# Two kinds of VectorE work put between the packed rows and their copy, and epsilon added by a sum over pairs

## The reference, cut to what matters

```python
def sm_attn(qq, kk, vv):
    s = scale * qq @ kk.T
    a = exp(s - max(s))
    a = a / (sum(a) + 1e-09)          # the epsilon of this case
    return a @ vv
packed = sm_attn(p, k, v)             # 32 rows per head
x = sm_attn(q, packed, packed)        # 576 tokens per head, over 32 packed rows
h = x @ w_in                          # 4608 tokens x 512 -> 1024
solu = h * softmax(h)
ln = (solu - mean) / sqrt(var + 1e-06) * g_ln
y = ln @ w_out                        # -> 512
h2 = max(y @ w1, y @ w2, y @ w3)      # -> 768
out = h2 @ w_out2                     # -> 512
```

## Time and profile before

| | |
|---|---|
| median of 3 runs | 1023.25 us |
| profiled execution, its own time | 1022.33 us |
| span from first to last instruction | 1020.5 us |
| TensorE busy | 993.5 us, 97% |
| VectorE busy | 594.0 us, 58% |
| ScalarE busy | 356.0 us, 35% |
| GpSimd busy | 269.4 us, 26% |
| mean granted TensorE clock | 0.998 of full speed |

### The profile page before, as it was taken

One profiled execution on the slowest core, in us unless ns is written; L12 is line 12 of the kernel. 1 busy time (PEld: TensorE's weight loads), 2 busy tenths in 40 slices (PEclk: granted clock), 3 DMA queues, 4 the chain that ended last, 5 costly groups with the idle time before them and its releaser, 6 DMA issues.

```text
span 1020.5 us, 14952 instructions
## 1 busy us (share of the span) xinstructions
PE 993.5 (97%) x6026; PEld 796.6 (78%) x6026; DVE 594.0 (58%) x960; ACT 356.0 (35%) x583; POOL 269.4 (26%) x228
## 2 busy tenths in 40 slices
PE   6989999999999999999999999999999999999998
PEld 5656567887887887878888888888888888888887
DVE  1788899765865767564655726664365736553121
ACT  5867753333442442333212422224122332122111
POOL 0368753439949992700000000000000000000000
PEclk9999999999999999999999999999999999999999
DMA  8979827226564582235745345453544535432341
GB/s 296 390 259 307 295 102 258 106 103 250 216 224 182 193 317 83 103 113 187 295 161 203 134 176 192 174 212 114 196 175 185 179 131 214 163 140 93 117 161 42
DMA packets 49764, 189.85 MB, mean 186 GB/s; under 512 B 9888, under 2 KB 9888, under 8 KB 39328
## 3 DMA queue, kind: packets, MB, share of 16 engines
q1 hardware_dynamic: 43472, 153.89, 42.4%
q0 software_dynamic: 6224, 35.00, 9.1%
HBM read 141.30 MB, written 47.58 MB: 185 GB/s over the span
## 4 chain that ended last, share of the span: by engine, by line
PE 84%; DVE 8%; ACT 4%; issue 3%; DMA 1%; POOL 0%; SPq 0%; ACTq 0%
PE ps L1171 28%; PE ps L783 27%; PE ps L1203 14%; PE ps L1194 5%; PE ps L1073 3%; PE ps L894 2%; DVE h_lo L1574 1%; PE ps L990 1%; DVE spot L1889 1%; PE ps L797 1%; DVE spot L1880 1%; DMA p_raw<-in_p_dram 1%; PE ps L799 1%; DVE a2T L1662 1%; ACT qT L1248 1%
## 5 line engine op out<-in xcount | busy, mean ns | idle before, releaser
L1171 PE MATMUL ps<-ys,slot 128*128 128x512 f32 x1512 | 345.8, 390 | 0.6
L1171 PEld LDWEIGHTS ps<-ys,slot 128*128 128x128 f32 x1512 | 283.2, 188 | 62.5 <-ACT spot L1248 4.0
L1880 DVE TENSOR_TENSOR spot<-ps,spot 128x512 f32<-128x512 f32 x108 | 74.3, 688 | 104.6 <-PE ps L1171 75.1
L1248 ACT ACTIVATE spot<-ps 128x512 f32<-128x512 f32 x90 | 52.8, 597 | 207.9 <-PE ps L1171 196.8
L783 PE MATMUL ps<-ln_lo,w_out_s_hi 128*128 128x512 f32 x280 | 109.2, 390 | 0.0
L783 PE MATMUL ps<-ln_hi,w_out_s_lo 128*128 128x512 f32 x280 | 109.0, 389 | 0.0
L783 PE MATMUL ps<-ln_hi,w_out_s_hi 128*128 128x512 f32 x280 | 108.9, 389 | 0.0
L1203 PE MATMUL ps<-w_out_s_lo,h_hi 128*128 128x512 f32 x216 | 84.0, 389 | 0.0
L1203 PE MATMUL ps<-w_out_s_hi,h_hi 128*128 128x512 f32 x216 | 84.0, 389 | 0.0
L1203 PE MATMUL ps<-w_out_s_hi,h_lo 128*128 128x512 f32 x216 | 84.0, 389 | 0.0
L1390 ACT ACTIVATE u<-ps,neg_max 128x1024 f32<-128x1024 f32 x36 | 40.2, 1117 | 112.7 <-DVE neg_max L1737 112.7
(11 more groups left out here) (160 smaller groups left out, 1504.0 us busy)
## 6 DMA issues: line engine op xcount, KB each, us to landing
slot<-w_operands SPq DMA_DIRECT2D x36, 1792.0 KB, 7.2
w_operands<-stage POOLq DMA_DIRECT2D x18, 1024.0 KB, 4.9
v_raw<-in_v_dram SPq DMA_DIRECT2D x8, 1152.0 KB, 7.1
q_raw<-in_q_dram SPq DMA_DIRECT2D x32, 288.0 KB, 5.3
y_features<-yst SPq DMA_DIRECT2D x9, 1024.0 KB, 4.8
y_raw<-y_features SPq DMA_DIRECT2D x9, 1024.0 KB, 5.2
out_dram<-spot SPq DMA_DIRECT2D x36, 256.0 KB, 2.0
slot<-w_operands SPq DMA_DIRECT2D x9, 1024.0 KB, 5.1
```

Source lines behind the costliest of these rows:

```text
L1171: last = pe.matmul(ps[:, group_bank(g, k), :], w[:, a - 1, i, kk, :], ys[:, b, j, kk, :], start=n < 4 and kk == 0 and e == 0, stop=kk == K ...
L1248: return act.activation(dst, src, ACT.Copy)
L1880: dve.tensor_tensor(dst[:, :], a, b, op).then_inc(ready, 1)
```

## The change

`sum1` and `sum2` get a second column that holds the epsilon, written once at the start; the row sums go to the first column, and the epsilon is added by a reduction over the pair instead of a tensor_scalar. `lo_a(b)` of batches 0 and 1 moves from the end of step b into step b+1, between `take_packed` and `copy_packedT`. The second `centre` of steps 3, 4 and 5 moves to the same place of its own step, ahead of `inverse2(b, 1)` and both `turn_out`.

```diff
-    sum1 = place("sum1", [P, QUADS])
+    sum1 = place("sum1", [P, QUADS, 2])
-    sum2 = place("sum2", [P, QUADS, S // NPACK])
+    sum2 = place("sum2", [P, QUADS, S // NPACK, 2])
+    eps_ready = sem("eps_ready")
...
-                               bias=nb1[:, g:g + 1], scale=SCALE, accum_out=sum1[:, g:g + 1]).then_inc(s1_exp, 1)
+                               bias=nb1[:, g:g + 1], scale=SCALE, accum_out=sum1[:, g, 0:1]).then_inc(s1_exp, 1)
...
             dve.memset(share[:, :], SHARE).then_inc(share_ready, 1)
+            dve.memset(sum1[:, :, 1], SM_EPS).then_inc(eps_ready, 1)
+            dve.memset(sum2[:, :, :, 1], SM_EPS).then_inc(eps_ready, 1)
+            dve.wait_ge(eps_ready, 2)
             dve.wait_ge(gain_loaded, 16)
...
                 dve.wait_ge(s1_exp, QUADS * b + QUADS)
-                dve.tensor_scalar(sum1_eps[:, :], sum1[:, :], SM_EPS, None, ALU.add).then_inc(inv1_step, 1)
+                dve.tensor_reduce(sum1_eps[:, :], sum1[:, :, :], AX.X, ALU.add).then_inc(inv1_step, 1)
...
-                dve.tensor_reduce(sum2[:, g, :], quad(g), AX.X, ALU.add).then_inc(inv2_step, 1)
+                dve.tensor_reduce(sum2[:, g, :, 0], quad(g), AX.X, ALU.add).then_inc(inv2_step, 1)
                 dve.wait_ge(inv2_step, c + 1)
-                dve.tensor_scalar(sum2_eps[:, g, :], sum2[:, g, :], SM_EPS, None, ALU.add).then_inc(inv2_step, 1)
+                dve.tensor_reduce(sum2_eps[:, g, :], sum2[:, g, :, :], AX.X, ALU.add).then_inc(inv2_step, 1)
...
             def step(b, third=True, second=True, first=True):
-                direct = third and b < 2
...
                 if second:
                     take_packed(b + 1)
+                if third and 0 < b < 3:
+                    lo_a(b - 1)
+                elif MEAN_STEP < b < B - 2:
+                    centre(b - MEAN_STEP - 1, 2 * (b - MEAN_STEP - 1) + 1)
                 if third and not first:
                     max_h(0, 1)
                 if second:
                     copy_packedT(b + 1)
...
-                if MEAN_STEP < b < B - 2:
-                    centre(b - MEAN_STEP - 1, 2 * (b - MEAN_STEP - 1) + 1)
                 if third:
                     turn_out(b, 1)
...
-                if direct:
-                    lo_a(b)
```

## The result

The changed kernel took 1017.07 us (median of 5 runs, 1016.94 to 1018.30) against 1022.72 us for the kernel before on the same chip (5 runs, 1021.96 to 1023.51): ratio 0.9950, 95% interval 0.9939 to 0.9962. On a second chip it was 1016.92 against 1023.25: 0.9943, 0.9930 to 0.9955. The forecast was 1017.8 (1016.2 to 1020.6), faster. Medians and intervals leave out two executions of the kernels of the experiments that took 2020.26 and 4927.88 us, far above their neighbours (one in part 2, one in part 3).

The account below looks back on a forecast made before the run. TensorE, busy 97%, was taken as the bound, so gains count only where it waits. Terms 0.67 + 2.20 + 1.30 - 0.68 + 0.41 + 0.33 + 0.26 + 0.93 = 5.42 us, from 1023.25 to 1017.8 (1016.2 to 1020.6).

Parts of the forecast that it names:

- lo_a(0), 0.67 of 1.26: End of step 0: moving it frees 1.26 us of VectorE's queue, of which 0.67 us reaches TensorE.
- lo_a(1), its wait and its hold: Step 2: GpSimd stretches lo_a(1) from 1.35 to 2.90 us; removing TensorE's wait for it brings another 2.20 us.
- The clock, 1.30: Step 2, turn_a1 to pack: with no idle time before, TensorE's half clock goes, another 1.30 us.
- the clock still falls: Rival, 8%: another idle time replaces the one removed, so the gain is 4.1 us, 1019.1 us.
- What is late next, -0.68: Step 2 into 3: GpSimd's backlog delays sub2(2, 0), exp2 and the kT copy for turn_q(3, 0); takes back 0.68 us.
- The new place: lo_a meets GpSimd's scale2: packed copy 0.40 us earlier in step 1, 1.36 us late in step 2 but covered.
- the rival of a partial loss: Rival, 22%: packed copies come later than worked out or step 2's cover shrinks; gain 3.0 us, 1020.2 us.
- the slower one: Rival, 4%: moved instructions queue behind GpSimd's scale2 and the packed copies behind them; 2.7 us slower, 1025.9 us.
- nothing arrives: Rival, 5%: DMA loads set the pace of the attention, steps lengthen at loads, up to the whole gain; 1023 us.
- centre, 0.41 + 0.26: Moving the second centre from between the two turn_out brings 0.41 us in step 3 and 0.26 in step 5.
- epsilon, 0.33 + 0.93: Adding the epsilon by an unheld reduction brings 0.33 us in step 5 and 0.93 in the last step.
- the prediction's sign: In the changed trace, TensorE's wait for u, before at 1.5 us in the last step, is 0.6 us.

Follow-up runs that it names:

- part 2: Against the kernel before: both moves with the epsilon still a tensor_scalar, 1020.49 us; lo_a's move and the epsilon change without centre's move, 1019.05 us.
- part 3: Changed kernel with lo_a and the second centre one place later, behind copy_packedT: 1021.08 us.
- experiment 4: Kernel before with GpSimd's batch-0 remainder held until lo_a(1) is done, 1022.72 us; kernel before with 18 extra TensorE transposes before scores2(2, 1), 1023.01 us.
- Experiment 5's first kernel: Changed kernel with GpSimd's split_merged(0, 1) behind both sub2 of batch 2 instead of in front: 1017.75 us.

## Why the prediction was right, step by step

**lo_a(0), 0.67 of 1.26.** Measured 0.68 and 0.64.

**lo_a(1), its wait and its hold.** `scores2(2, 1)` was forecast 2.87 us earlier by the ruler and came so: 61.12 - 0.56 (the start) - 2.87 = 57.69, measured 57.70. That the hold by GpSimd is what made 1.35 into 2.90 is shown by experiment 4.

**The clock, 1.30.** `turn_a1` to `pack` is 2.09 as forecast, and `pack` 65.19 - 0.56 - 60.47 = 4.16 us earlier (4.17). So 1.30 is right for the place. What it is worth further on is less, and the prediction's own bounds say so: with the half clock kept, `pack`, and `turn_q(3, 0)` behind it, would be 2.87 us earlier, against 3.49 with GpSimd's bound. Within this change the clock then brings 0.62 us (an estimate, from these two bounds), since the other 0.68 is what the backlog takes back. So the rival "the clock still falls", for a fall at this place, was priced 0.7 us too high. In the kernel before the traces give 0.91 at the end (experiment 4), but the executions don't confirm it: the mean granted clock of before was 0.998 in 53 of 63, median 1023.31, and 0.999 or 1.000 in 6, median 1022.40, and these six spread from 1022.02 to 1024.60. By its mean granted clock 1 execution of before in 10 doesn't have the fall that the one trace showed.

**What is late next, -0.68.** `sub2(2, 0)` 60.75 (forecast 60.81, the start taken off), `turn_q(3, 0)` 63.17 (63.28). Experiment 5's first kernel gives 0.63 back when the backlog is moved: its `turn_q(3, 0)` is 4.17 us earlier, as much as the prediction had for `pack`.

**The new place.** The packed copy of step 2 was to be 1.36 us late: it starts at 66.32, and TensorE had been ready at 64.96 (the `turn_packed` of 64.48 takes 0.44), 1.36. Its cover held. The copies behind `centre`, VectorE in steps 3, 4 and 5:

```profile
81.53 0.74 DVE L1590 SCALAR_TENSOR_TENSOR weight_raw<-w_out_raw,gain,column_mean 128x512 f32<-128x512 f32 x1
82.91 0.58 DVE L1631 COPY packedT<-ps 64x128 f32<-64x128 f32 x2 [0.65 <-PE ps L905]
...
96.94 1.00 DVE L1590 SCALAR_TENSOR_TENSOR weight_raw<-w_out_raw,gain,column_mean 128x512 f32<-128x512 f32 x1
98.32 0.58 DVE L1631 COPY packedT<-ps 64x128 f32<-64x128 f32 x2 [0.39 <-PE ps L905]
...
111.97 1.07 DVE L1590 SCALAR_TENSOR_TENSOR weight_raw<-w_out_raw,gain,column_mean 128x512 f32<-128x512 f32 x1
113.36 0.58 DVE L1631 COPY packedT<-ps 64x128 f32<-64x128 f32 x2 [0.32 <-PE ps L905]
```

VectorE still idles 0.65, 0.39 and 0.32 us in front of each copy (forecast 0.6, 0.2, 0.1), so the rival of a partial loss did not occur, nor the slower one, which needs copies late by more than the hole in most of the five steps. For "nothing arrives", a load would have to hold TensorE; none of its waits from 26 to 147 us names one.

**centre, 0.41 + 0.26; epsilon, 0.33 + 0.93.** The first and the last are confirmed one by one: 0.41 in the table at b=5, 0.40 against the kernel without `centre`'s move; 0.91 to 0.94 for the wait for `u`, which is 0.6 us in the kernel run again, as the prediction's sign had it. The two of step 5 add up (0.59 forecast; from b=5 to b=7 the table gives 0.50 and 0.65), but their division was wrong: alone, the epsilon brings 0.03 there, and taking `centre`'s move out of the whole costs 0.60 there and 1.28 in all, not 0.67. That the two sizes of step 5 made up for each other is luck.

**The sentence that failed.** "What the freed stalls are worth: step 3 (0.6) and step 4 (0.7) nothing" is right against the kernel before, and wrong as a price of the edit. It took the stalls of before as given, and didn't ask where the tensor_scalars would stand once the moves had shifted VectorE against GpSimd: 2.12 us in step 3. Without the epsilon's change about 3 of 5.6 us would have been lost again. The sum came out right because it was made for all the parts together.

**The clock in step 7.** The prediction held 1.79 us of idle time to be harmless, since before has such a one with no fall behind it. In the changed kernel's trace:

```profile
136.42 0.27 PE L839 MATMUL ps<-qT,packedT 64*32 64x64 f32 x5 [1.78 <-ACT qT L1249]
...
138.61 1.76 PE L1074 MATMUL ps<-ident,u 128*128 128x128 f32 x8
```

and in the same kernel run again:

```profile
136.27 0.27 PE L839 MATMUL ps<-qT,packedT 64*32 64x64 f32 x5 [1.79 <-ACT qT L1249]
...
137.60 1.09 PE L1074 MATMUL ps<-ident,u 128*128 128x128 f32 x8
```

Eight transposes take 1.76 us behind one and 1.09 behind the other. So the rival "the clock still falls" does occur, elsewhere and in some executions, for 0.75 us. Part of what the slower matmuls take falls into a wait that was there: TensorE's 0.6 us for `u`, which the kernel run again has, is absent in the execution with the fall. By the mean granted clock 2 of 10 executions of the changed kernel have a fall (0.998), too few to move the median.

## What to carry to other kernels

Price several edits of one queue together and in shifted times: here an addition over two elements, worth 0.9 us alone, decided about 3 us of 5.6 (by the ruler). When VectorE is moved against GpSimd, look for every small tensor_scalar, of two elements per partition or more, that will now start inside one of GpSimd's two-input instructions, and make it a reduction if it can be one. Work moved off a path is cheap only in a hole that the engine has anyway; one place later the same instructions cost 3.3 us by the ruler.

## What was not expected of the hardware

**How long GpSimd holds VectorE depends on GpSimd's instruction.** Its two-input TENSOR_TENSOR holds to its end (the rows above). Its one-input TENSOR_SCALAR of 2.77 us holds only at first. GpSimd in step 3 of the changed kernel:

```profile
80.55 2.76 POOL L692 TENSOR_SCALAR m_odd<-merged_first 128x1024 fp32r<-128x1024 f32 x1
```

`centre`, two inputs in SBUF, starts 0.98 us later at 81.53 and takes its normal 0.74. GpSimd in the kernel with both moves:

```profile
58.46 2.77 POOL L691 TENSOR_SCALAR m_even<-merged_first 128x1024 fp32r<-128x1024 f32 x1
```

and VectorE beside it:

```profile
58.55 0.97 DVE L1599 TENSOR_SCALAR sum_eps<-sum 128x2 f32<-128x2 f32 x1 [0.55 <-ACT a L1277]
```

58.55 + 0.97 = 59.52, 1.06 us behind GpSimd's start and 1.71 ahead of its end. The 0.46 us of the earlier trace rows ends at 150.08, 1.07 behind the start of this one in the kernel before:

```profile
149.01 2.77 POOL L658 TENSOR_SCALAR w_out_s_hi<-weight_raw 128x1024 fp32r<-128x1024 f32 x1 [0.64 <-DVE weight_raw L1586]
```

The unheld 1.19 us of the earlier trace rows began 1.64 us into its like the earlier trace rows. So it is about the first microsecond that holds; why, no run here shows.

The whole-length rule weighed in the prediction (the Trainium skill, "SBUF — State Buffer", Who interferes with whom) thus holds for GpSimd's two-input instructions and not for this one, and its 1.0 us in step 3 was not paid. The same section of the Trainium skill says that tensor_reduce never contends for the shared port pair on this chip, while tensor_scalar can. With that the trace agrees: 24 reductions between 156 and 193 ns, none held.

**A tensor_scalar with one element per partition is not held.** The additions that were held have 2 and 18. The one behind each row maximum has one, and this one of the kernel before starts 0.61 us into the GpSimd instruction of 56.70 to 59.06:

```profile
57.31 0.15 DVE L1594 TENSOR_SCALAR nb<-m 128x1 f32<-128x1 f32 x1
```

All 14 of them take 153 to 156 ns. The `lo_a(1)` right behind it, at 57.38, is the one that took 2.90 in place of 1.35 us.

**A clock that falls by chance.** In the profiled executions without added transposes, TensorE's clock went from 1.00 to 0.50 behind 2.2 us of idle time in step 2 in all three kernels that have it (before, and two of the parts alone), and behind 1.78 to 1.88 us in step 7 in 2 of 11. By the ruler one fall costs 0.7 to 0.9 us at the end (0.91 in step 2, 0.75 and 0.66 in step 7). A single profile can't tell whether every execution pays it; the mean granted clock of each execution (53 of 63 at 0.998 for before, 7 of 10 at 1.000 for the changed kernel) tells that most of one kernel's do and most of the other's don't.
